# Clustered attention and two MLPs in one kernel: clusters of one pair of heads at a time, chosen amid attention

## Chip, cores and metric

One core of a Trainium2 chip runs the whole program. The metric is the device time of one execution in microseconds (us). Engines: TensorE (PE, its weight loads PEld), VectorE (DVE), ScalarE (ACT), GpSimd (POOL); SyncE (SP) and ACT issue DMAs.

## What is computed

```python
q_n, k_n, c_n = q / |q|, k / |k|, centroids / |centroids|     # (2, 8, 768, 64) and 8 heads x 16 clusters
q_assign = argmax(q_n @ c_n.T); k_assign = argmax(k_n @ c_n.T)   # first of equal maxima
mask = q_assign[..., :, None] == k_assign[..., None, :]
attn = softmax(where(mask, q @ k.T / 8, -1e9)) @ v
x = attn, heads side by side                                   # (1536, 512)
h = x @ w_in; g = h * sigmoid(1.702 * h); x = g @ w_out        # width 2048
h = x @ w_in2; s = h * softmax(h); x = layernorm(s) * g_ln @ w_out2   # width 1024
```

Length of q and k does not change an argmax, so only the centroids are normalized. The mask comes into the scores as 16 more rows of the contraction: a one-hot row set for q, and one times -2^100 for k, so that a query whose cluster differs from the key's gets a large negative term.

## The kernel before

Each engine has its own program; the order of its work is written by hand, and semaphores join the programs.

**Clusters** are found first, in 8 lots (2 batches x q or k x 2 halves of the 768 tokens, each lot all 8 heads). Per lot: `sims_of` (L446, four matmuls 128x32 weights by 384 columns, L453), `copy_sims` on ACT (L705), three transposes (`tokens_of`, L465), on DVE a maximum over 16 clusters and a comparison (`compare`, L919 and L921), on POOL a product with a falling rank, so that the first of equal maxima wins (`rank_lot`, L1244), and on DVE a second maximum and comparison (`choose`, L930 and L935). Two lots make one set of one-hot rows: six transposes back (`hots_of`, L476) and an ACT copy to `hot_t` (`store_clusters`, L715), which goes by DMA to `mask_rows` in HBM (L368, L719). Six lots are chosen and two sets turned back before attention; the rest falls into its first steps (`HOT_STEPS`, `STORE_STEPS`, `CHOOSE_STEPS`, L261).

**Attention** runs over 8 pairs of heads (`it`), 12 steps each (`n`, 6 tiles of 128 queries for each head of the pair). `place_head` (L323, SP) moves halves of a head's split k and q and its cluster rows (L336, two DMAs of 48 KB) into the tiles that scores read. Step n:

- PE: turn the probabilities of step n-6 (`turn`, L519, 6 transposes), scores of step n (`scores_of`, L502 and L506), and a part of a half head (`head_half`, L534: 12 matmuls per 3 steps, in parts of 3, 5 and 4; part 0 and 1 behind the scores, part 2 before them).
- ACT: copy of the turned halves (`turned_high`, L772, two), the exponential (`exps`, L761), and in some steps k_high (L728), a copy of the half head (`x_of_low_v`, L778) or xh (L784).
- DVE: row maximum (L959), two small ones on sums in even steps (L967, L973), `x_sum` (L986) every third step, `turned_low` (L979, two).
- POOL: scaling of probabilities (L1221), k_low (L1158) and splits of v and x.

The order of a step on PE and DVE, and the banks (PSUM has 8):

```python
TURN_LAG, HEAD_LAG, X_LAG = 5, 6, 9
def pt_bank(step, c): return banks[:, 4 + (2 * step + c) % 3, 0:HALF]   # turned halves: 3 banks in turn
head_out = banks[:, 7, 0:HALF]                                          # one bank for all half heads
pe.wait_ge(pt_low_done, 2 * g - 2 + c)                                  # turn, half c of turn g
if exists(it, n, CH, STEPS): pe.wait_ge(x_done, it * 4 + half)          # head_half, part 0
```

Scores use banks 0 to 3. The pair `it` = 0 is written out, the others are loops with register operands on all engines (`Fori`). Behind attention come the first MLP (PE L549 to L566), and the second (L639 to L672), which the change leaves alone.

Of the kernel before, what the change touches and what calls it, by code (L numbers as in the profile page):

```python
# [5 lines left out]
ALU = mybir.AluOpType  # L6
# [6 lines left out]
P = 128  # L13
# [3 lines left out]
def clustered_attention_two_mlps(nc, q_t, k_t, v_r, cent, w_gelu, w_ln, gains, out):  # L17
# [24 lines left out]
    assert HC == P and DM == BANK and QT % 2 == 0 and F2 == 2 * BANK and UNITS == 16  # L42
# [3 lines left out]
    mask_rows = nc.dram_tensor("mask_rows", (2, B, HC, S), F32, kind="Internal").ap()  # L46
    mask_heads = mask_rows.rearrange("x b (h c) s -> x (b h) c s", c=C)

    with ExitStack() as ctx:
# [26 lines left out]
        pair_t = [sb(f"pair_t{x}", [P, HP, S], F32, raw34, "right") for x in range(2)]  # L76
        sims_t = [sb(f"sims_t{x}", [P, S], F32, raw34, "right") for x in range(2)]
        raw34.close()
# [3 lines left out]
        first_rank_i = sb("first_rank_i", [P, C], I32, cluster)  # L82
        first_rank = sb("first_rank", [P, C], F32, cluster)
# [5 lines left out]
        LOTS = 4 * B  # L89
        CHOICE_LAG = 1  # L90
        RANKS = CHOICE_LAG + 2
        sims_max = [sb(f"sims_max{r}", [P, CH * H], F32, cluster) for r in range(RANKS)]
        rank_max = [sb(f"rank_max{r}", [P, CH * H], F32, cluster) for r in range(RANKS)]
        rank = [sb(f"rank{r}", [P, HALF], F32, cluster) for r in range(RANKS)]
        hot = [sb(f"hot{x}", [P, S], F32, cluster) for x in range(2)]
        hot_t = [sb(f"hot_t{x}", [P, S], F32, cluster) for x in range(2)]
# [47 lines left out]
        sims_t_ps = [banks[:, 2 * x:2 * x + 2, 0:HALF] for x in range(2)]  # L144
        sims = [banks[:, 4 + c, 0:HALF] for c in range(2)]
        hot_ps = banks[:, 6:8, 0:HALF]
# [3 lines left out]
        def pt_bank(step, c):  # L150
            return banks[:, 4 + (2 * step + c) % 3, 0:HALF]

        head_out = banks[:, 7, 0:HALF]
# [18 lines left out]
        pair_loaded = [two_sems(f"pair_loaded{x}_") for x in range(2)]  # L172
# [5 lines left out]
        ranked = sem("ranked")  # L178
        rank_max_done = sem("rank_max_done")
        hot_done = sem("hot_done")  # L180
        hot_ps_done = sem("hot_ps_done")
        hot_t_done = sem("hot_t_done")
        mask_stored = two_sems("mask_stored")
# [68 lines left out]
        TURN_LAG, HEAD_LAG, X_LAG = 5, 6, 9  # L252
# [8 lines left out]
        KQ_STEP, STORE_STEPS, HOT_STEPS, CHOOSE_STEPS = 0, (2, 4), (3, 5), (0, 1)  # L261
# [27 lines left out]
        def _(sp):  # L289
            sp.dma_start(c_raw[:], cent).then_inc(cent_loaded, 16)  # L290
            sp.dma_start(gains_sb[:], gains).then_inc(gains_loaded, 16)


            def load_pairs(e):
                b, x, c = e // 4, e // 2 % 2, e % 2
                if b > 0:

                    sp.wait_ge(sims_t_done, e - 3)
                half = slice(c * HALF, (c + 1) * HALF)
                sp.dma_start(pair_t[x][:, :, half], (q_pairs, k_pairs)[x][b][:, :, half]  # L300
                             ).then_inc(pair_loaded[x][c], 16)
# [21 lines left out]
            def place_head(it, j):  # L323
# [6 lines left out]
                def cluster_rows(dst, x):  # L330
                    src = mask_heads[x, bass.ds(h, 1)].rearrange("o c s -> (o c) s")
                    if isinstance(it, int) and it == 0 and j == 0:

                        sp.wait_ge(hot_t_done, x + 1)
                        src = hot_t[x][0:C, :]
                    sp.dma_start(dst.bitcast(F32), src).then_inc(qk_ready[j], 16)  # L336
# [4 lines left out]
                if isinstance(it, int) and it == 0 and j == 0:  # L341

                    load_pairs(LOTS - 1)
# [5 lines left out]

                sp.wait_ge(low_moved[j], (it + 1) * 16)  # L350
                for x, rows in enumerate((q_high[j], k_low[j])):
                    cluster_rows(rows[D:AUG, :], x)
# [13 lines left out]
            for x in range(2):  # L366
                sp.wait_ge(hot_t_done, x + 1)
                sp.dma_start(mask_rows[x, 0], hot_t[x][:]).then_inc(mask_stored[x], 16)  # L368
            for j in range(2):
                load_v(0, j)  # L370
            load_kq(1, 0)

            for x in range(2):
                sp.wait_ge(mask_stored[x], 16)
            place_head(0, 1)

            def place_turn(it, last=False):
                load_kq(it, 1)
                place_head(it, 0)
                load_v(it, 0)  # L380
                if not last:
                    load_kq(it + 1, 0)
                place_head(it, 1)
                load_v(it, 1)
                load_ln(it)


            sp.wait_ge(sims_done, LOTS)
            load_ln(0)

            for x in range(2):
                sp.wait_ge(mask_stored[x], 16 * B)
            with sp.Fori(1, ITS - 1) as it:
                place_turn(it)
            place_turn(ITS - 1, last=True)


# [40 lines left out]
        def _(pe):  # L438

            pe.wait_ge(gpsimd_consts, 4)  # L440
# [5 lines left out]
            def sims_of(e):  # L446
                b, x, c = e // 4, e // 2 % 2, e % 2
                pe.wait_ge(pair_loaded[x][c], (b + 1) * 16)
                if e >= 4:

                    pe.wait_ge(sims_t_copied, e - 3)
                for n in range(HP):
                    last = nc.tensor.matmul(sims_t_ps[x][n * 2 * C:(n + 1) * 2 * C, c, :], c_diag[:, n, :],  # L453
                                            pair_t[x][:, n, c * HALF:(c + 1) * HALF], start=True, stop=True)
                last.then_inc(sims_t_done, 1)

            def tokens_of(e):
                x, c = e // 2 % 2, e % 2
                pe.wait_ge(sims_t_copied, e + 1)
                if e >= 2:  # L460

                    pe.wait_ge(compared, e - 1)
                for i in range(CH):
                    t = c * CH + i
                    last = nc.tensor.transpose(sims[c][:, i * P:(i + 1) * P], sims_t[x][:, t * P:(t + 1) * P],  # L465
                                               ident[:])
                last.then_inc(sims_done, 1)


            def hots_of(g):  # L470
                pe.wait_ge(hot_done, (g + 1) * 2)
                if g >= 1:

                    pe.wait_ge(hot_t_done, g)
                for i in range(QT):
                    last = nc.tensor.transpose(hot_ps[:, i // CH, i % CH * P:(i % CH + 1) * P],  # L476
                                               hot[g % 2][:, i * P:(i + 1) * P], ident[:])
                last.then_inc(hot_ps_done, 1)

            for e in range(4):  # L480
                sims_of(e)
                if e >= 1:
                    tokens_of(e - 1)
# [836 lines left out]
```

## Time and profile before

| | |
|---|---|
| runs | 671.86, 672.01, 675.32 us (median 672.01) |
| profiled execution | 672.1 us, span 670.3 us, granted clock 0.986 |
| clusters until the first scores | 0 to 31.5 us |
| attention, pair 0 | 31.5 to about 58 us |
| attention, pairs 1 to 7 | 27.0 us each, to about 247 us |
| drain and first MLP | to about 540 us |
| second MLP | to 670 us |

The span is from the first to the last instruction; 1.8 us of the time lie around it. Engine rows give busy time; matmuls overlap, so a busy PE need not be at its peak. In a timeline an idle time in brackets stands with what ended it; the chain of waits is followed back from the last instruction, and "issue" in it is time for which the profile shows no wait.

### The profile page before, as it was taken

How to read it: one execution, taken by the hardware profiler on the slowest of the kernel's cores; microseconds unless marked ns; L12 is line 12 of the kernel's file. 1: busy time of each engine (PE TensorE's matmuls, PEld its weight loads, DVE VectorE, ACT ScalarE, POOL GpSimd, SP SyncE). 2: the span in 40 equal slices, each digit the busy share in tenths (PEclk: the TensorE clock that was granted, in tenths of full speed). 3: DMA queues.
4: the chain of work that ended last, by engine and by line, in shares of the span. 5: the costliest groups of instructions: out<-in, count | busy, mean ns of one | idle time of the engine just before them, and what ended most of it. 6: DMA issues, size and time to landing. Idle time of an engine off the chain costs nothing.

```text
span 670.3 us, 11572 instructions
## 1 busy us (share of the span) xinstructions
PE 639.0 (95%) x3281; PEld 537.8 (80%) x3281; DVE 434.5 (65%) x759; ACT 321.0 (48%) x641; POOL 419.7 (63%) x590
## 2 busy tenths in 40 slices
PE   5689999999999999999999999999999999999998
PEld 1369989898989888788877888788888878888886
DVE  3779999999999985666657667562222554545352
ACT  1279999999999984222232222132222243324232
POOL 2677788798888886888878888878886100000000
PEclk9779999999999999999999999999999999999999
DMA  8866544544544421232222222222231022112101
GB/s 284 245 185 154 159 120 112 143 122 126 143 112 137 130 92 64 72 113 87 104 94 93 90 99 94 94 95 94 94 106 51 29 82 77 52 60 78 63 16 47
DMA packets 39601, 70.52 MB, mean 105 GB/s; under 512 B 4256, under 2 KB 22688, under 8 KB 39584
## 3 DMA queue, kind: packets, MB, share of 16 engines
q1 hardware_dynamic: 37568, 66.38, 33.1%
q10 hardware_dynamic: 2016, 3.93, 1.6%
q8 instruction: 8, 0.13, 0.1%
q14 instruction: 9, 0.07, 0.0%
HBM read 46.60 MB, written 4.72 MB: 77 GB/s over the span
## 4 chain that ended last, share of the span: by engine, by line
PE 68%; ACT 10%; issue 9%; DVE 5%; DMA 4%; POOL 2%; DVEq 1%; SPq 1%; ACTq 0%; POOLq 0%
PE banks L534 6%; PE banks L549 6%; PE banks L551 6%; PE banks L550 6%; PE banks L564 6%; PE banks L566 6%; PE banks L565 5%; PE banks L639 5%; ACT probs L761 4%; PE banks L519 4%; PE banks L672 3%; PE banks L671 3%; PE banks L670 3%; ACT probs_th L772 3%; PE banks L642 2%
## 5 line engine op out<-in xcount | busy, mean ns | idle before, releaser
L979 DVE TENSOR_TENSOR probs_tl<-banks,probs_th 128x384 fp32r<-128x384 f32 x192 | 100.5, 547 | 11.7 <-ACT probs_th L772 9.4
L959 DVE TENSOR_REDUCE neg_max<-banks 128x1 f32<-128x768 f32 x96 | 91.3, 951 | 8.6 <-PE banks L506 6.6
L772 ACT CAST probs_th<-banks 128x384 fp32r<-128x384 f32 x192 | 83.0, 485 | 20.8 <-PE banks L519 19.5
L761 ACT ACTIVATE probs<-banks,neg_max 128x768 f32<-128x768 f32 x96 | 88.3, 920 | 7.1 <-DVE neg_max L959 7.0
L953 DVE TENSOR_TENSOR gl<-gate,gh 128x512 fp32r<-128x512 f32 x48 | 48.2, 1003 | 66.8 <-ACT gh L746 66.8
L1145 POOL TENSOR_TENSOR wait_scrap<-half_power 128x1 f32<-128x1 f32 x176 | 46.4, 264 | 67.1 <-PE banks L566 33.7
L1221 POOL TENSOR_SCALAR probs<-probs,row_inv 128x768 f32<-128x768 f32 x96 | 87.0, 907 | 0.0
L1284 POOL TENSOR_TENSOR stat<-stat,half_power 128x1 f32<-128x1 f32 x12 | 6.6, 549 | 127.5 <-DVE stat L1092 127.5
L519 PE MATMUL banks<-ident,probs 128*128 128x128 f32 x576 | 79.0, 273 | 1.3 <-ACT hot_t L715 1.3
L534 PE MATMUL banks<-probs_th,v_parts 128*128 128x384 f32 x192 | 70.4, 367 | 9.8 <-DVE x_sums L986 9.8
L746 ACT CAST gh<-gate 128x512 fp32r<-128x512 f32 x48 | 29.8, 621 | 101.1 <-PE banks L566 52.7
L549 PE MATMUL banks<-xh,uph 128*128 (+1 forms) x192 | 76.0, 396 | 0.4 <-POOL upl L1194 0.4
L564 PE MATMUL banks<-gh,downh 128*128 128x512 f32 x192 | 75.8, 395 | 0.2
L566 PE MATMUL banks<-gh,downl 128*128 128x512 f32 x192 | 75.3, 392 | 0.0
L551 PE MATMUL banks<-xh,upl 128*128 (+1 forms) x192 | 75.3, 392 | 0.0
L550 PE MATMUL banks<-xl,uph 128*128 (+1 forms) x192 | 75.1, 391 | 0.0
L565 PE MATMUL banks<-gl,downh 128*128 128x512 f32 x192 | 74.8, 390 | 0.0
L1204 POOL TENSOR_TENSOR downl<-gelu_raw,downh 128x512 fp32r<-128x512 f32 x48 | 71.4, 1488 | 4.0
L519 PEld LDWEIGHTS banks<-ident,probs 128*128 128x128 f32 x576 | 68.5, 140 | 5.7 <-ACT hot_t L715 1.6
L742 ACT ACTIVATE gate<-banks 128x512 f32<-128x512 f32 x48 | 28.7, 599 | 81.8 <-PE banks L551 57.0
L1194 POOL TENSOR_TENSOR upl<-gelu_raw,uph 128x512 fp32r<-128x512 f32 x48 | 62.7, 1306 | 4.0
L534 PE MATMUL banks<-probs_tl,v_parts 128*128 128x384 f32 x192 | 65.1, 339 | 0.0
(100 smaller groups left out, 1346.1 us busy)
## 6 DMA issues: line engine op xcount, KB each, us to landing
gelu_raw<-w_gelu SPq DMA_DIRECT2D x48, 512.0 KB, 3.3
ln_raw<-w_ln SPq DMA_DIRECT2D x8, 512.0 KB, 4.3
pair_t<-q_t SPq DMA_DIRECT2D x4, 768.0 KB, 7.3
pair_t<-k_t SPq DMA_DIRECT2D x4, 768.0 KB, 8.2
kq_raw<-k_t SPq DMA_DIRECT2D x16, 192.0 KB, 3.5
kq_raw<-q_t SPq DMA_DIRECT2D x16, 192.0 KB, 3.7
q_parts<-k_high SPq DMA_DIRECT2D x16, 192.0 KB, 2.6
q_high<-k_high SPq DMA_DIRECT2D x16, 192.0 KB, 3.0
```

Source lines behind the costliest of these rows:

```text
L519: last = nc.tensor.transpose(pt_bank(n, c)[:, t * P:(t + 1) * P], probs[:, n % NP, k * P:(k + 1) * P], ident[:])
L534: last = nc.tensor.matmul(head_out, v_parts[j][:, i // 2].rearrange("p two d -> p (two d)"), part[half % 2][:, i // 2, :], start=i == 0, s ...
L549: nc.tensor.matmul(hidden[u], uph[u][:, cols], xh[:, k, tok], start=k == 0, stop=False)
L550: nc.tensor.matmul(hidden[u], uph[u][:, cols], xl[:, k, tok], start=False, stop=False)
L551: last = nc.tensor.matmul(hidden[u], upl[u][:, cols], xh[:, k, tok], start=False, stop=k == KT - 1)
L564: nc.tensor.matmul(acc[d], downh[u][:, cols], gh[u][:], start=first, stop=False)
L565: nc.tensor.matmul(acc[d], downh[u][:, cols], gl[u][:], start=False, stop=False)
L566: last = nc.tensor.matmul(acc[d], downl[u][:, cols], gh[u][:], start=False, stop=end)
L761: nc.scalar.activation(probs[:, n % NP, :].rearrange("p (c t) -> p c t", c=2), scores[n % 2], ACT.Exp, bias=neg_max[:, n % NP:n % NP + 1], ...
L772: nc.scalar.copy(probs_th[half % 2][:, c * CH:(c + 1) * CH, i * P:(i + 1) * P], pt_bank(n, c).rearrange("p (t s) -> p t s", t=CH)).then_in ...
L959: nc.vector.tensor_reduce(out=neg_max[:, col], in_=scores[n % 2], op=ALU.max, axis=mybir.AxisListType.XY, negate=True).then_inc(max_done, 1)
L979: nc.vector.tensor_tensor(probs_tl[half % 2][at], pt_bank(n, c).rearrange("p (t s) -> p t s", t=CH), probs_th[half % 2][at].bitcast(F32), ...
```

## The change

There are 8 lots, one for each pair of heads: q and k, both halves of the tokens, in one matmul group of the same shape as before (4 x 2C rows). Lot 0 is made whole before attention, lot 1 half; its rest lies in steps 1 and 3 of pair 0. Lot e >= 2 lies in the 12 steps of pair e-2: sims at step 1, its transposes and `compare` at step 4, transposes back and `copy_ties` at step 7, the tie matmul and `choose` at step 10. POOL ranks nothing any more: a 128x128 matrix `first_w` (made once on POOL with two `affine_select` and two subtractions) is multiplied with the transposed comparison, and `choose` is one comparison of the product, from PSUM to `hot_t`. Nothing goes through HBM: `cluster_rows` is four DMAs of 24 KB per head out of `hot_t`.

The lots borrow the banks of the half heads (6 and 7; lot 1 uses 4 and 5). Turned halves get two banks in place of three, half heads two in place of one, with later waits; `X_LAG` is 10. `x_of_low_v` goes to the head of a step, ahead of `turned_high`, and so from steps 1, 4, 7, 10 to 2, 5, 8, 11; xh from 6 and 9 to 7 and 10. `gains` is loaded later. All attention loops are written out (`for` in place of `Fori`).

```diff
-        TURN_LAG, HEAD_LAG, X_LAG = 5, 6, 9
+        TURN_LAG, HEAD_LAG, X_LAG = 5, 6, 10
+        LOT_LEAD = 2
+        LOT_STEPS = [{"sims_t": 1, "sims": 4, "ties": 7, "first": 10}] * (LOTS - LOT_LEAD)
-            return banks[:, 4 + (2 * step + c) % 3, 0:HALF]
-        head_out = banks[:, 7, 0:HALF]
+        def pt_bank(c):
+            return banks[:, 4 + c, 0:HALF]
+        def head_out(half):
+            return banks[:, 6 + half % 2, 0:HALF]
+        LOT_UNITS = ("sims_t", "sims", "ties", "first")
+        def lot_bank(what, e):
+            w = LOT_UNITS.index(what) % 2
+            return banks[:, (5 - w if e == 1 else 6 + w), 0:HALF]
@@ SP
-                    sp.dma_start(dst.bitcast(F32), src).then_inc(qk_ready[j], 16)
+                def cluster_rows(rows, x):
+                    for c in range(2):
+                        at = (x * 2 + c) * 2 * C + j * C
+                        sp.dma_start(rows[D:AUG, c * HALF:(c + 1) * HALF].bitcast(F32), hot_t[it % 2][at:at + C, :]
+                                     ).then_inc(qk_ready[j], 16)
-            for e in range(4):
-                load_pairs(e)
+            load_pair(0)
             load_kq(0, 0)
-            for e in range(4, LOTS - 1):
-                load_pairs(e)
+            load_pair(1)
             load_kq(0, 1)
+            sp.dma_start(gains_sb[:], gains).then_inc(gains_loaded, 16)
             place_head(0, 0)
...
@@ PE
+            def sims_of(e):
+                for x in range(2):
+                    for c in range(2):
+                        n = x * 2 + c
+                        last = nc.tensor.matmul(dst[n * 2 * C:(n + 1) * 2 * C, :], c_diag[:, e % HP, :],
+                                                pair_t[x][:, e % 2, c * HALF:(c + 1) * HALF], start=True, stop=True)
+            def first_of(e):
...
+                nc.tensor.matmul(lot_bank("first", e), first_w[:], ties_t[:], start=True, stop=True
+                                 ).then_inc(first_done, 1)
-                    if exists(it, n, 2 - c, STEPS):
-                        pe.wait_ge(pt_low_done, 2 * g - 2 + c)
+                    if g >= 1:
+                        pe.wait_ge(pt_low_done, 2 * g - 1 + c)
-                    if exists(it, n, CH, STEPS):
-                        pe.wait_ge(x_done, it * 4 + half)
+                    if exists(it, n, 2 * CH, STEPS):
+                        pe.wait_ge(x_done, it * 4 + half - 1)
+                    read, count = lot_read(it * 4 + half)
+                    pe.wait_ge(read, count)
+                    if not drain:
+                        for what, of in zip(LOT_UNITS, (sims_of, tokens_of, ties_of, first_of)):
+                            for e in lot_at(it, n, what):
+                                of(e)
-            attention_turn(0)
-            with pe.Fori(1, ITS) as it:
+            for it in range(ITS):
                 attention_turn(it)
@@ ACT
+            def copy_ties(e):
+                act.wait_ge(ties_done, e + 1)
...
+                nc.scalar.copy(ties_t[:], lot_bank("ties", e)).then_inc(ties_t_copied, 1)
@@ DVE
+                nc.vector.tensor_tensor(heads(ties[:]), sim, sims_max[:].unsqueeze(2).to_broadcast([P, G, C]), ALU.is_ge
...
+                nc.vector.tensor_scalar(hot_t[e % 2][:], lot_bank("first", e), hot_from[:], hot_scale[:], ALU.is_ge,
+                                        ALU.mult).then_inc(hot_t_done, 1)
@@ POOL
-            X_SPLIT_STEPS = [QT + 3, QT + 4]
+            X_SPLIT_STEPS = [QT + 2, QT + 5]
-            for e in range(LOTS):
-                rank_lot(e)
+            scale_q(0, 0)
+            first_weights()
```

## Rows read from the trace of the kernel before

**Rows 1.** Busy time by stretch: us, PE, PEld, DVE, ACT, POOL, clock, DMA share, GB/s
```profile
0.00:31.50 31.50, 18.27 (x102) 6.78 (x102) 18.27 (x39) 7.37 (x12) 13.45 (x23) 0.88 0.85 260
31.50:45.70 14.20, 11.05 (x42) 9.34 (x42) 9.50 (x17) 8.37 (x16) 9.82 (x14) 0.66 0.82 229
...
99.50:126.50 27.00, 25.74 (x170) 24.04 (x169) 25.43 (x53) 24.93 (x58) 22.88 (x35) 1.00 0.48 129
```

**Rows 2.** Waits, 100 to 225 us: us in total, times, longest
```profile
PEld banks L534 <- DVE x_sums L986: 11.4, 18, 0.7
```

**Rows 3.** Chain of waits, 98 to 129 us: start, us, what
```profile
110.80 0.48 ACT x_sums L778
...
111.82 0.56 DVE x_sums L986
```

**Rows 4.** Timeline of PEld, 104 to 113 us: start, us, what
```profile
106.08 0.76 PEld L519 LDWEIGHTS banks<-ident,probs 128*128 128x128 f32 x6
...
108.31 0.75 PEld L519 LDWEIGHTS banks<-ident,probs 128*128 128x128 f32 x6
...
110.38 0.75 PEld L519 LDWEIGHTS banks<-ident,probs 128*128 128x128 f32 x6
...
112.43 0.19 PEld L534 LDWEIGHTS banks<-probs_th,v_parts 128*128 128x128 f32 x1 [0.68 <-DVE x_sums L986]
```

**Rows 5.** Timeline of ACT, 46 to 52 us, pair 0, two exponentials in a row
```profile
49.64 0.90 ACT L761 ACTIVATE probs<-banks,neg_max 128x768 f32<-128x768 f32 x1
...
51.43 0.90 ACT L761 ACTIVATE probs<-banks,neg_max 128x768 f32<-128x768 f32 x1
```

**Rows 6.** Timeline of DVE, 49 to 59 us, pair 0, three row maxima in a row
```profile
50.44 0.95 DVE L959 TENSOR_REDUCE neg_max<-banks 128x1 f32<-128x768 f32 x1
...
52.36 0.95 DVE L959 TENSOR_REDUCE neg_max<-banks 128x1 f32<-128x768 f32 x1
...
54.15 0.95 DVE L959 TENSOR_REDUCE neg_max<-banks 128x1 f32<-128x768 f32 x1
```

**Rows 7.** Timeline of ACT, 98 to 114 us, k_high and what follows it
```profile
99.42 0.84 ACT L728 CAST k_high<-kq_raw 128x768 fp32r<-128x768 f32 x1
100.15 0.88 ACT L772 CAST probs_th<-banks 128x384 fp32r<-128x384 f32 x2
```

**Rows 8.** Groups of instructions, 0 to 36 us: busy us, mean ns | idle before
```profile
L921 DVE TENSOR_TENSOR rank<-banks,sims_max 128x384 f32<-128x384 f32 x8 | 4.5, 558 | 0.3
L919 DVE TENSOR_REDUCE sims_max<-banks 128x24 f32<-128x384 f32 x8 | 4.4, 551 | 9.1 <-PE banks L465 9.1
L705 ACT COPY sims_t<-banks 128x384 f32<-128x384 f32 x8 | 3.8, 478 | 16.3 <-PE banks L453 16.3
...
L1158 POOL TENSOR_TENSOR k_low<-kq_raw,k_high 128x384 fp32r<-128x384 f32 x2 | 2.6, 1314 | 0.0
```

**Rows 9.** Timeline of PEld and PE, 22 to 26 us: a lot's matmuls behind transposes
```profile
24.35 0.16 PEld L453 LDWEIGHTS banks<-pair_t,c_diag 128*32 128x32 f32 x8 [0.17 <-issue]
...
24.35 0.85 PE L453 MATMUL banks<-pair_t,c_diag 128*32 128x384 f32 x8
```

**Rows 10.** Chain of waits over the span, first part: start, us, what
```profile
8.31 1.50 PE banks L453 x8
9.82 0.83 PE banks L465 x3
...
22.87 5.32 DMA q_parts<-k_low
...
28.83 2.62 DMA k_low<-hot_t
```

**Rows 11.** Timeline, 0 to 22 us: the first lot
```profile
6.30 1.51 PE L453 MATMUL banks<-pair_t,c_diag 128*32 128x384 f32 x8 [1.57 <-DMA pair_t<-q_t]
```

**Rows 12.** Timeline, 22 to 60 us: second head of pair 0
```profile
35.14 0.82 ACT L728 CAST k_high<-kq_raw 128x768 fp32r<-128x768 f32 x1
...
45.71 0.30 PEld L502 LDWEIGHTS banks<-k_high,q_parts 128*128 128x128 f32 x2 [1.25 <-DMA k_low<-mask_rows]
```

More of the change, by code:

```diff
@@ L384, in place_turn @@
                 load_v(it, 1)
+                if it + 3 < LOTS:
+                    load_pair(it + 3)
                 load_ln(it)
[L388 to L395, printed above, removed]
+            for j in range(2):
+                sp.wait_ge(qk_ready[j], READY * ITS)
             def gelu_turn(it):
@@ L438, in _ @@
         def _(pe):
[L440 removed]
+            pe.wait_ge(gpsimd_consts, 3)
             pe.wait_ge(cent_unit_done, 1)
@@ L446, in sims_of @@
             def sims_of(e):
[L447 to L454, printed above, removed]
+                pe.wait_ge(pair_loaded[e % 2], (e // 2 + 1) * 32)
@@ L802, in attention_turn @@
                             kq_high(0, 1)
-                        if n in STORE_STEPS:
-                            store_clusters(2 + STORE_STEPS.index(n))
+                    if not drain:
+                        for what, of in (("sims_t", copy_sims), ("ties", copy_ties)):
+                            for e in lot_at(it, n, what):
+                                of(e)
                     if drain and n in GATE_STEPS:
                         gelu(0, GATE_STEPS.index(n))
-            attention_turn(0)
-            with act.Fori(1, ITS - 1) as it:
-                attention_turn(it)
-            attention_turn(ITS - 1, last=True)
+            for it in range(ITS):
+                attention_turn(it, last=it == ITS - 1)
             attention_turn(ITS, X_STEPS[-1] + 1, drain=True)
@@ L939, in _ @@
-            for b in range(B):
-                for e in range(4 + CHOICE_LAG):
-                    if e < 4:
-                        compare(b * 4 + e)
-                    if e >= CHOICE_LAG and b * 4 + e - CHOICE_LAG < LOTS - len(CHOOSE_STEPS):
-                        choose(b * 4 + e - CHOICE_LAG)
+                dve.wait_ge(first_done, e + 1)
+                if e == 0:
+                    dve.wait_ge(hot_consts, 4)
+                if e >= 2:
+                    for j in range(2):
+                        dve.wait_ge(qk_ready[j], READY * (e - 1))
@@ L1007, in attention_turn @@
                         turned_low(*lagged(it, n, TURN_LAG, STEPS), 1)
+                    if not drain:
+                        for what, of in (("sims", compare), ("first", choose)):
+                            for e in lot_at(it, n, what):
+                                of(e)
                     if drain and n in GATE_STEPS:
@@ L1011, in _ @@
             dve.wait_ge(guard_set, 1)
-            attention_turn(0)
-            with dve.Fori(1, ITS) as it:
+            for it in range(ITS):
                 attention_turn(it)
```

299 lines of the change are left out of this document (137 added, 162 removed).

## The prediction

> **What bounds the kernel now.** I read the busy table by stretch first, since clusters, attention and MLPs have different limits. [rows 1] show three stretches that the change touches: 31.5 us until the first scores, 14.2 us from there to the scores of the second head, and laps of 27.0 us for a pair. In a lap PE is busy 25.7 us, DVE 25.4 and ACT 24.9, so no engine has much room, and what ends a wait decides. The waits say which: PE's weight loads stood 11.4 us in 18 waits, all for x_sum [rows 2], and 125 us are 4.63 laps, so 2.5 us a lap, four waits of 0.6. The chain shows the loop behind it: the half head's copy on ACT, x_sum on DVE, then the next half head on PE [rows 3, 4]. There is one bank for half heads, so each must be emptied before the next begins.
>
> In the first stretch the chain [rows 10] runs over DMAs: moving k_low took 5.3 us among the big pair loads, the cluster rows 2.6 more.
>
> **Part 1, up to the first scores.** All 8 lots' loads stood in front; now only 0.79 MB (pair 0's q and k) come first. The first load landed at 6.3 us before [rows 11], itself 0.79 MB; I take 6.0. Then at the slow clock: sims 1.5, copy 0.5, transposes 0.8, compare 1.15, transposes 0.8, copy 0.5, tie matmul 0.5 (one matmul of their 384 columns, between one transpose's 0.3 and the 0.8 of all three), choose 0.56 [rows 8, 10, 11]: 12.3 us. Choose has no row: a plain comparison of its size took 0.56 [rows 8]; its bounds are 0.48, a copy's, and 1.1, compare's two together.
>
> Beside it k and q of head 0 land at about 7.5 (1.18 MB at 260 GB/s, [rows 1], behind an issue at 1.2, plus the landing); scaling and k_high end near 10. On POOL `first_weights` now stands ahead of k_low: four operations of 128 columns or less, for which no row stands; by width a third of k_low's 1.3 [rows 8] is 0.45 each, 1.8 in all; between nothing and 4 x 1.3 = 5.2. With 1.2 to 1.8 and two k_low of 1.3, k_low is ready at about 12.9. Its move takes 2.6 to 5.3 [rows 10]; the pair loads are then through, so 2.6: 15.5. SP then issues two DMAs of cluster rows, 0.6, and they land 2.6 later: first scores at 18.7, against 31.5. Gain 12.8, between 10 and 14.
>
> **Part 2, second head of pair 0.** Its k_high comes behind the first exponential on ACT, as before, at 35.14, and the scores waited for the cluster rows until 45.71 [rows 12]: 10.6 us for k_low, moves and rows. That order stays; what goes is the store to HBM and back and the DMA load of the other lots, what comes is two more issues on SP. I take 9.3, gain 1.3, between -1 and 3.
>
> **Part 3, cost of a lot in a lap.** PE: sims, of the shape they had, took 0.85 at the fast clock, with 0.17 idle ahead [rows 9]: 1.02 in step 1. Three transposes at half of six's 0.7 [rows 4] are 0.35 in step 4 and in step 7; the tie matmul is taken at 0.18, half of those, in step 10. Sum 1.9. The 0.17 is a row: weight loads of 32 columns waited for transposes of 128, and nothing is named but issue. The Trainium skill (TensorEngine Tiling (Array Packing), Key Properties) says that a change of tiling mode drains TensorE. The row agrees. A lot changes the mode twice; by this rule 0.17 more would be paid on the way back, 1 us over six lots. ACT: two copies of 0.48 [rows 8], steps 1 and 7. DVE: compare 1.15 in step 4, choose 0.56 in step 10.
>
> **Part 4, the lap.** Step lengths of one engine without waits: ACT 1.79 [rows 5]; DVE 1.79, and 1.92 in even steps [rows 6]; PE 2.23, 2.07 and, less its stall of 0.68, about 1.9 [rows 4]. Extras: k_high 0.73 [rows 7], a half-head copy or an xh 0.48, x_sum 0.5 [rows 3]. Sums over 12 steps before: PE 24.8, DVE 24.2, ACT 25.8. Taking the longest engine in each step and adding gives 27.3, and the lap took 27.0: steps are coupled nearly rigidly.
>
> After, PE has 26.7, DVE 25.9, ACT 26.8: no lap with a lot can be under 26.8. The longest engine per step, 0 to 11, is 2.4 (DVE), 3.25 (PE), 2.3, 2.3, 3.1 (DVE with compare), 3.0 (ACT: k_high and the half-head copy now meet in 5 and 11), 2.4, 2.75 (ACT), 2.3, 2.3, 2.5, 3.0: 31.5. That is the upper bound. Two banks for turned halves make PE's turn wait for DVE's `turned_low` of the turn just before. That loop takes turn 0.7, copy 0.5, subtraction 0.55, about 1.75, so a step forgives some 0.4 us. Walking turn by turn with this (turn begins at the latest of PE's own step, and 1.05 behind the ACT copy's start; the copy at the latest of turn plus 0.5 to 0.7, and ACT's last work; DVE in its order) puts the turns of steps 0 to 12 at 0, 1.9, 5.1, 7.2, 9.4, 12.0, 14.0, 16.7, 19.3, 21.4, 24.0, 26.4, 28.5, and the lap carries 0.4 into the next: 28.9. Without a lot the same walk gives 26.3: the old wait on x_sum goes, but ACT's 25.8 is close behind.
>
> Who waits behind the new waits: in steps 3, 6, 9 and 0 part 0 of a half head stands on PE until the lot has left its bank; the walk has the lot out 0.2 to 0.6 us ahead. Compare delays row maximum 5 and so exponential 5; late next is ACT.
>
> At nothing: pair loads amid attention (DMA share 0.48 a lap [rows 1], some 0.6 after), four more small issues on SP a lap, `gains`. If that cover were gone, scores would wait at steps 0 and 6. The written-out loops I also take at nothing.
>
> **Sum**, against the profiled execution's 672.1 (the median is the same within 0.1): -12.8 - 1.3; pair 0's lots 1 and 2 among its steps +1.1; pairs 1 to 5, 5 x (28.9 - 27.0) = +9.5; pairs 6 and 7, 2 x (26.3 - 27.0) = -1.4; x_sum one step later in the drain +0.3. Together -4.6: 667.5 us.
>
> **Rivals.**
> (a) *The lots hide in the old stall.* The stall of 2.5 us a lap was as large as PE's 1.9, and ACT and DVE have the room by their sums. Laps of 27.0 with a lot, 25.9 without: -12.8 - 1.3 + 0.5 - 2.2 + 0.3 gives 656.6. For it: every sum is under 27. Against it: steps 1, 4, 5 and 11 each load one engine 3 us, and two banks leave little to even that out.
> (b) *Slower: the two-bank loop holds the steps rigidly.* The place is PE's turn waiting for `turned_low`, above all behind compare and sims. The lap then nears 31.5, and gain and loss meet where it is 27.0 + 14.1 / 5 = 29.8. At 30.5 with 27.5 for pairs 6 and 7 it gives -12.8 - 1.3 + 1.6 + 17.5 + 1 + 0.3: 678.4. For it: 27.3 against 27.0 before, though then with three banks. Against it: the 0.4 us of slack.
> (c) *Pair 0 runs late.* The clock was 0.66 between the first scores and the second head's [rows 1], at times at 1.2 GHz, and PE has less to do ahead of scores now; a slow clock for some 6 us more in full steps costs 3, a late second head 1 to 2: 671.5.
> (d) *It doesn't remove what it seems to:* the half-head bank was one of two equal waits, so pairs 6 and 7 stay at 27.0. That is +1.4, 669, and stands in (c)'s range.
>
> **Numbers.** Forecast 0.40, (a) 0.23, (b) 0.19, (c) and (d) 0.18. This kernel's measurement tells about 0.5% (3.4 us) from nothing. Faster by more than that (under 668.6): a good half of the forecast, 0.26, all of (a), 0.03 of (c) and (d): 0.52. Slower (over 675.4): most of (b), 0.18, and 0.02 of (c): 0.20. The same: 0.28. The range 656 to 678 takes in (a) and the lower half of (b).
>
> **What would show it.** First scores at 18 to 20 us; second head's some 13 us behind them; laps with a lot of 28.2 to 29.6 and without of 26 to 26.6; in place of PE waiting for x_sum, PE at L519 waiting for `turned_low`, most in steps 2 to 3 and 6 to 7. It is wrong if laps 1 to 5 stay near 27, if they pass 30, or if first scores come after 21.

## The result, and the profile after

| | before | after |
|---|---|---|
| runs, median | 671.93 us (671.83 to 675.32) | 676.91 us (676.27 to 677.69) |
| profiled execution, span | 672.1, 670.3 us | 677.22, 675.5 us |
| first scores | 31.50 us | 17.96 us |
| first scores of the second head, behind the first | 14.2 | 12.35 |
| first scores of pair 1, behind those | 11.8 | 16.22 |
| laps of pairs 1 to 5 | 26.42, then 27.0 to 27.2 | 30.65, then 29.58 four times |
| lap of pair 6 (no lot) | 27.00 | 27.10 |
| pair 7 to the first matmul of the MLP | 31.88 | 32.18 |
| from there to the end | 419.2 | 420.7 |

The ratio is 1.0066, 95% interval 1.0039 to 1.0093: slower, if by little. 15.4 us came in until the second head and 20.6 us went out behind it. The same table of stretches as [rows 1], of the kernel after:

```profile
0.00:17.96 17.96, 6.73 (x27) 2.36 (x27) 4.44 (x19) 3.55 (x5) 6.77 (x20) 1.00 0.68 184
17.96:30.31 12.35, 9.87 (x45) 7.45 (x45) 7.12 (x13) 7.04 (x15) 6.37 (x10) 1.00 0.69 184
30.31:46.53 16.22, 12.09 (x77) 10.30 (x77) 13.42 (x28) 13.90 (x31) 13.55 (x21) 1.00 0.67 174
46.53:52.00 5.47, 5.47 (x26) 5.13 (x30) 3.62 (x7) 1.85 (x4) 2.11 (x4) 0.69 0.65 177
77.20:106.80 29.60, 27.82 (x187) 24.74 (x184) 26.83 (x57) 26.02 (x59) 22.94 (x35) 1.00 0.57 145
195.50:222.60 27.10, 26.48 (x171) 23.74 (x170) 25.67 (x54) 25.34 (x57) 22.97 (x35) 1.00 0.45 115
```

The clock column is not to be read before 24.1 us: the profile has no clock record there, and the durations say that PE was slow (sims took 1.51 at 21.3 us and 0.85 in the laps; the first scores 1.01, those at 26.65 us 0.62).

A lap with a lot keeps PE busy 27.8 us of 29.6, one without 26.5 of 27.1. The waits between 100 and 225 us show that the wait for x_sum of [rows 2] is gone, and which waits stand now:

```profile
ACT probs_th L778 <- PE banks L534: 10.9, 16, 0.9
DVE probs_tl L978 <- ACT probs_th L778: 7.9, 15, 0.8
PE banks L534 <- DVE probs_tl L978: 6.8, 16, 0.7
```

L534 is now the turn, L778 its copy on ACT, L978 the subtraction on DVE (`turned_low`). Beside them PE's weight loads stand 14.3 us ahead of turns, and the profile names no wait for that. PE, ACT and DVE stand for one another in turn: a ring in which the work of each comes behind that of the last. The chain of waits through a lap with a lot (pair 2; start, us, what) goes round it:

```profile
80.56 0.89 PE banks L551 x5
81.45 0.78 PE banks L458 x8
...
84.50 0.37 ACT sims_t L719
...
84.89 0.26 ACT x_sums L784
...
85.39 0.49 ACT probs_th L778
...
85.90 0.57 DVE probs_tl L978
...
86.60 0.98 PE banks L534 x6
...
89.16 0.33 PE banks L469 x3
...
91.45 0.47 DVE sims_max L921
...
91.95 0.56 DVE ties L926
92.50 0.87 DVE neg_max L958
...
96.50 0.33 PE banks L479 x3
...
99.35 0.30 ACT ties_t L727
```

Every piece of the lot but choose stands in this chain: sims 0.78 and its copy 0.37, transposes 0.33, compare 1.03, transposes 0.33, copy 0.30, and the tie matmul (0.17, at 104.02). That is 3.3 us, and the lap is 2.5 longer than one without a lot: some of it is covered, and a piece in the chain is not yet a price.

**Ahead of pair 1** the loss has another cause. SP's timeline there, with PE's below it:

```profile
29.67 0.43 SPq L314 DMA_DIRECT2D pair_t<-q_t  x1
30.14 0.43 SPq L314 DMA_DIRECT2D pair_t<-k_t  x1
30.62 0.43 SPq L367 DMA_DIRECT2D ln_raw<-w_ln  x1
31.09 0.51 SPq L324 DMA_DIRECT2D kq_raw<-k_t  x1
31.65 0.60 SPq L324 DMA_DIRECT2D kq_raw<-q_t  x1
32.57 0.90 SPq L342 DMA_DIRECT2D q_parts<-k_high  x1
33.51 0.70 SPq L342 DMA_DIRECT2D q_high<-k_high  x1
35.74 0.46 SPq L342 DMA_DIRECT2D q_parts<-k_low  x1
42.17 0.46 SPq L342 DMA_DIRECT2D k_high<-k_high  x1
```

```profile
46.53 0.62 PE L515 MATMUL banks<-k_high,q_parts 128*128 128x384 f32 x2 [3.53 <-DMA k_low<-hot_t]
...
48.93 0.99 PE L515 MATMUL banks<-k_high,q_parts 128*128 128x384 f32 x2
```

Within 2.6 us SP issued a pair load, the `ln` load and k and q of the next head, 1.66 MB, and right behind them pair 1's moves of k_high. Those were issued at 32.6 and 33.5 and landed 7.4 and 8.6 us later, and SP's next step, which waits for them, came at 42.17. PE stood 3.5 us for the cluster rows behind it. 1.4 us after it had started again it fell to 1.2 GHz for 3.4 us: the same scores take 0.99 in place of 0.62, and the granted clock is 0.69 from 46.5 to 52.0. The Trainium skill (DMA: Bandwidth & Descriptors, Queues, rings and completion order) says that each DMA engine takes a queue's descriptors in ring order; moves issued behind 1.66 MB of loads landed 8.6 us behind their issue here in place of 3.0, which agrees.

### The profile page after: what moved, and what is told of

Read it like the earlier page. It is cut to its first block, busy times and chain, and to the rows that moved or that the text cites. A ratio compares the mean times of both kernels' runs of the same rounds, so it can differ in the third digit from the quotient of the medians.

```text
span 675.5 us, 10622 instructions
## 1 busy us (share of the span) xinstructions
PE 641.4 (95%) x3289; PEld 535.7 (79%) x3289; DVE 424.8 (63%) x754; ACT 323.0 (48%) x645; POOL 412.3 (61%) x586
## 4 chain that ended last, share of the span: by engine, by line
PE 74%; ACT 8%; DVE 7%; issue 5%; DMA 2%; POOL 2%; SPq 1%; POOLq 0%; DVEq 0%; ACTq 0%
PE banks L534 7%; PE banks L566 6%; PE banks L654 6%; PE banks L568 6%; PE banks L581 6%; PE banks L567 6%; PE banks L583 6%; PE banks L582 6%; PE banks L551 5%; PE banks L686 3%; PE banks L687 3%; PE banks L685 3%; ACT probs_th L778 3%; DVE probs_tl L978 3%; PE banks L657 3%
## 5 line engine op out<-in xcount | busy, mean ns | idle before, releaser
L978 DVE TENSOR_TENSOR probs_tl<-banks,probs_th 128x384 fp32r<-128x384 f32 x192 | 100.6, 548 | 20.6 <-ACT probs_th L778 19.5
L778 ACT CAST probs_th<-banks 128x384 fp32r<-128x384 f32 x192 | 85.0, 483 | 30.3 <-PE banks L534 29.2
L534 PE MATMUL banks<-ident,probs 128*128 128x128 f32 x576 | 85.8, 282 | 11.8 <-DVE probs_tl L978 11.5
L534 PEld LDWEIGHTS banks<-ident,probs 128*128 128x128 f32 x576 | 63.9, 141 | 33.8 <-issue 25.2
L952 DVE TENSOR_TENSOR gl<-gate,gh 128x512 fp32r<-128x512 f32 x48 | 46.1, 960 | 69.6 <-ACT gh L752 69.6
L752 ACT CAST gh<-gate 128x512 fp32r<-128x512 f32 x48 | 29.8, 621 | 102.2 <-PE banks L583 57.4
L551 PE MATMUL banks<-probs_th,v_parts 128*128 128x384 f32 x192 | 67.9, 353 | 0.0
```

What stands on the lines that cost most here:

```text
L534: last = nc.tensor.transpose(dst[:, t * P:(t + 1) * P], probs[:, n % NP, k * P:(k + 1) * P], ident[:])
L551: last = nc.tensor.matmul(head_out(half), v_parts[j][:, i // 2].rearrange("p two d -> p (two d)"), part[half % 2][:, i // 2, :], start=i = ...
L778: nc.scalar.copy(probs_th[half % 2][:, c * CH:(c + 1) * CH, i * P:(i + 1) * P], pt_bank(c).rearrange("p (t s) -> p t s", t=CH)).then_inc(p ...
L978: nc.vector.tensor_tensor(probs_tl[half % 2][at], pt_bank(c).rearrange("p (t s) -> p t s", t=CH), probs_th[half % 2][at].bitcast(F32), ALU ...
```

## Experiments

Each is one run, and stands beside runs of the kernel before (medians of 672.9 to 673.7 us, where the result above has 671.93) unless an interval is given; so I read laps first, and the whole time only where it moves by more than 2 us. "Later loads" is `new_loads_later` below, from which most of the later kernels start.

**1. Where the bound lay before.** Three parts of the change alone, or undone.

`old_written_out`: the loops alone, on all five engines.

```diff
-            with pe.Fori(1, ITS) as it:
+            for it in range(1, ITS):
```

> The kernel before with its attention loops written out, nothing else. Theory (loops cost nothing): laps stay at 27.0 us, time 672 within 1. Rival (branches and register waits cost): laps 26.5 or less, time under 668. Other rival (code loading costs in straight code): over 674.

672.21 us, laps 27.01 to 27.03. Writing the loops out costs and gives nothing.

`old_two_two`: the same, with the change's banks.

```diff
-            return banks[:, 4 + (2 * step + c) % 3, 0:HALF]
-
-        head_out = banks[:, 7, 0:HALF]
+            return banks[:, 4 + c, 0:HALF]
+
+        def head_out(half):
+            return banks[:, 6 + half % 2, 0:HALF]
...
-                    if exists(it, n, 2 - c, STEPS):
-                        pe.wait_ge(pt_low_done, 2 * g - 2 + c)
+                    if exists(it, n, 1, STEPS):
+                        pe.wait_ge(pt_low_done, 2 * g - 1 + c)
...
-                    if exists(it, n, CH, STEPS):
+                    if exists(it, n, 2 * CH, STEPS):
...
-                        pe.wait_ge(x_done, it * 4 + half)
+                        pe.wait_ge(x_done, it * 4 + half - 1)
```

> The kernel before, written out, with two banks for turned halves and two for half heads, the order of work unchanged (X_LAG 9, half-head copy behind the exponential). Theory 1 (the bank split only moves the wait from x_sum to turned_low): laps 26.8 to 27.3. Theory 2 (it is the new place of the half-head copy that holds the pairs without a lot at 27.1; the split by itself frees the wait): laps 25.8 to 26.5, time 664 to 668.

673.49 us, laps 27.20: theory 1. PE's wait for x_sum is gone. In the kernel before it had two rows between 100 and 225 us, the weight loads' in [rows 2] (11.4 us) and the matmuls' own, half as long, since matmuls are still at work while the next weights wait:

```profile
PE banks L534 <- DVE x_sums L986: 5.7, 18, 0.4
```

In `old_two_two` this stands in its place:

```profile
PE banks L520 <- DVE probs_tl L980: 6.2, 18, 0.5
```

The wait has moved, the lap has not shrunk. And PE never stood 2.5 us a lap: 5.7 us in 4.63 laps are 1.2. The last of this group takes only the part that can hurt, two banks for turned halves and still one for half heads:

`old_two_one`: of the diff above only `pt_bank` and the wait for `pt_low_done`.

> The kernel before with written-out loops (672.21 us, laps 27.0), two banks in turn for turned halves in place of three, and still one for half heads: the half of the bank split that can cost. Theory G (give and take: the second half-head bank gives what the missing third turned bank takes, which is why the lap without a lot stayed at 27.1 where a gain was forecast): without the second half-head bank both waits stand, PE for x_sum before part 0 and PE for turned_low one step later; laps 27.6 to 28.6, 677 to 683 us. Theory E (the engines' own work sets 27.0, banks of either kind don't matter): 27.0 to 27.3, 672 to 674 us.

Laps 27.28. In all 678.33 us, a time of G's range and not of E's, but its first scores came at 33.6, 2.1 later than before, and pair 0 took 1.0 more; only the laps are read. By them theory E's number holds, and G, on which I had come to rely, falls. Its two waits do not even add up: PE stands for x_sum as before, and for `turned_low` only weight loads stand, 0.8 us in all.

```profile
PE banks L534 <- DVE x_sums L986: 6.3, 18, 0.4
```

With or without either bank, a lap without a lot takes 27.0 to 27.3, and PE stands 1.2 to 1.4 us in it.

**2. Pair 1.** `new_loads_later`: the kernel after with two loads later.

```diff
             load_v(0, 1)
-            load_pair(3)
-            load_ln(0)
             for it in range(1, ITS):
                 load_kq(it, 1)
                 place_head(it, 0)
                 load_v(it, 0)
+                if it == 1:
+                    load_pair(3)
+                    load_ln(0)
```

> The changed kernel with pair 3's load and the first weight load of the second MLP issued behind the moves of head 0 of pair 1. Theory 1 (1.3 MB of loads ahead of those moves made them late and PE stood 3.5 us before pair 1, then ran at half clock): scores of pair 1 begin at 43 or earlier in place of 46.5, time 672 to 674. Theory 2 (ACT and POOL are late with k_high and k_low for that head): the wait stays, time 676 to 677.

671.74 us: pair 1's first scores stood 11.8 behind the second head's, as before the change. Its lap 1 was still 30.66: PE waited 0.66 us for the pair load that is now issued later (sims in step 1), and its weight loads 0.35 and 0.55 for the cluster rows of the next two heads. The same edit with an interval, as `new_loads_timed`:

> The kernel after with nothing but the two loads moved behind pair 1's first moves, against before with an interval: 670.5 to 673.5 us, ratio 0.997 to 1.001. Against after's 676.9 that is the 5 us which stood in PE's wait for the cluster rows and the slow clock behind it; if it is over 675, the one look was luck and the loads are not the cause.

Here lap 1 was 29.37, and the clock stayed at 1.00 from 23.5 us on. 672.32 us (671.06 to 673.69, 9 runs), 0.998 of before, 95% interval 0.9969 to 0.9991. Its SP timeline has the k_high moves landed by 36.07, 3.2 us behind their issue:

```profile
32.92 0.60 SPq L342 DMA_DIRECT2D q_high<-k_high  x1
35.56 0.46 SPq L342 DMA_DIRECT2D q_parts<-k_low  x1
36.07 0.60 SPq L342 DMA_DIRECT2D k_high<-k_high  x1
```

So the change's net loss lay in the place of 1.28 MB of loads. What is left is a balance near zero: 15 us gained ahead, 13 lost in laps 1 to 5, the rest in the last two pairs and the drain.

**3. What a lot costs in a lap.** All but `new_x_behind` on top of the later loads (laps 29.57, and 27.10 without a lot).

`new_one_sim`:

```diff
                         n = x * 2 + c
+                        if e >= LOT_LEAD and n != 3:
+                            continue
```

> The kernel after with the later loads; of the four sims matmuls of each lot from the third on, only the last is left (the other rows of the lot are not computed). PE gets 0.6 us less in step 1. Theory R: in step 1 PE's own work (turn, scores, five matmuls of the half head, sims) is the longest path round, so the whole 0.6 comes off the lap: 28.9 to 29.0. Theory S as well for this step. If the lap stays at 29.4 or more, the turn behind sims waits for DVE anyway and PE's extra work is not what a lot costs; then 671 us. With the 0.6: 668.4 to 668.9 us.

672.02 us, laps 29.52, where 668.4 to 668.9 and 28.9 to 29.0 were expected. The expectation was wrong about PE: one matmul took as long as four. The sims in this kernel, and in the kernel after:

```profile
105.86 0.83 PE L461 MATMUL banks<-pair_t,c_diag 128*32 128x384 f32 x2
```
```profile
110.96 0.85 PE L458 MATMUL banks<-pair_t,c_diag 128*32 128x384 f32 x8
```

The four go to four different groups of 32 columns, and 0.85 for four beside 0.83 for one says that they run side by side. The Trainium skill (TensorEngine Tiling (Array Packing), Key Properties) says that different tiles can execute in parallel; these rows agree.

`new_no_sims`: all four left out.

```diff
                             for e in lot_at(it, n, what):
-                                of(e)
+                                if what != "sims_t":
+                                    of(e)
...
-                act.wait_ge(sims_t_done, e + 1)
+                act.wait_ge(sims_t_done, min(e + 1, LOT_LEAD))
```

> The kernel after with the later loads; all four sims matmuls of each lot from the third on are left out (the copy takes what stands in the bank, so these lots are not computed). One matmul or four took the same time on PE, 0.85, since the four go to different columns of the array side by side; so the run that left one in took away nothing. Theory P (in steps 1 and 2 PE has no idle time, its own work is the path): with none left step 1 is shorter by the 0.74 between sims and the turn behind them and by the 0.17 to 0.25 of idle time ahead: 3.0 to 3.2 in place of 3.94, laps with a lot 28.6 to 28.8, 666.5 to 668 us. Theory D (DVE or ACT hold step 1): laps above 29.3, 671 us or more.

668.29 us; in the steady laps step 1 takes 3.22 in place of 3.94 to 3.97, as it does without a lot, and step 3 2.45 in place of 2.50; laps 28.78. Theory P.

`new_no_compare`: the same on DVE.

```diff
-                pe.wait_ge(compared, e + 1)
+                pe.wait_ge(compared, min(e + 1, LOT_LEAD))
...
-                                of(e)
+                                if what != "sims" or e < LOT_LEAD:
+                                    of(e)
```

> The kernel after with the later loads; DVE's compare (maximum and comparison, 1.03 us) is left out of each lot from the third on, so these lots turn back the comparison of an earlier one. Theory R: compare stands in front of row maximum 5, so it comes off almost whole, less what PE's transposes of the lot in step 4 hold: laps 28.7 to 29.0, 667.5 to 669 us. Theory S (PE is the bound behind step 4): 29.3 or more, 670.5 to 671.5 us. With the one sim of the run before this splits the 2.5 us of a lot; what is left over by both, 0.8 to 1, is the transposes, the copies and choose.

667.92 us; step 6 2.07 in place of 2.71, no other changed, laps 28.90 to 28.93. Theory R. The two prices, 0.79 and 0.66, are those of the two pieces alone; compare itself lasts 1.03, so 0.37 of it was covered. From the steps' lengths (with a lot less without) the rest is 0.42 in step 3, 0.30 in step 4 and 0.38 in step 9. By their place these are the sims' copy, the transposes and the ties' copy, but no run took them out one by one. Together 2.5; nothing is left for choose.

`new_x_behind`: the half head's copy on ACT behind the exponential of the step before, as it had been, on top of the kernel after (676.91 us, laps 29.58).

```diff
-TURN_LAG, HEAD_LAG, X_LAG = 5, 6, 10
+TURN_LAG, HEAD_LAG, X_LAG = 5, 6, 9
...
-                        x_of_low_v(*lagged(it, n, X_LAG - 1, STEPS))
...
                     if not drain:
                         exps(it, n)
...
+                        x_of_low_v(*lagged(it, n, X_LAG - 1, STEPS))
```

> The changed kernel with the half-head copy back behind the exponential (steps 1, 4, 7, 10) and X_LAG 9. Theory 1 (the copy ahead of turned_high stands in the loop turn, ACT copy, subtraction, turn, and costs 0.3 to 0.5 each): laps with a lot 28.0 to 28.8 in place of 29.6, pair 6 26.3 or less, the drain 1 us shorter, time 669 to 673. Theory 2 (the lot's work sets the lap): laps 29.4 to 29.7, time 675 to 677.

679.67 us, laps 30.23 to 30.30 with a lot, 27.61 without, against both theories: the new place is the better one. Most of the loss stands in step 6, 3.42 in place of 2.71, where PE waited 1.3 us for `turned_low` and its weight loads for POOL's scaled probabilities. Why these came late there stays open. The next moves the other end of the half head, x_sum on DVE.

`new_x_sum_last`:

```diff
-                        x_sum(*lagged(it, n, X_LAG, STEPS))
...
                         turned_low(*lagged(it, n, TURN_LAG, STEPS), 0)
...
                         turned_low(*lagged(it, n, TURN_LAG, STEPS), 1)
...
+                        x_sum(*lagged(it, n, X_LAG, STEPS))
```

> The kernel after with the later loads (671.74 us, laps with a lot 29.57, without 27.10) and on DVE x_sum moved behind both turned_low of its step. Theory R (a ring: turn and scores on PE, row maximum and then turned_low on DVE, and only then the next turn; what stands on DVE between row maximum and turned_low counts whole): the step that follows each x_sum (steps 0, 3, 6, 9 hold one, 0.5 us each) gets up to 0.5 shorter where PE had waited for turned_low 0.3 to 0.65; laps with a lot 28.2 to 28.8, without 26.0 to 26.6, in all 663 to 666 us. Theory S (the engines' own work in a step sets it, DVE has the same work wherever x_sum stands): laps 29.4 to 29.7 and 27.0 to 27.2, 671.5 us.

687.59 us, laps 32.5 with a lot and 27.84 without: my largest miss, of the wrong sign. PE in step 1:

```profile
113.11 0.85 PE L459 MATMUL banks<-pair_t,c_diag 128*32 128x384 f32 x8 [0.86 <-DVE x_sums L987]
```

The lot's pieces live in the half heads' banks. A piece can't start until x_sum has emptied the bank, and all that stands behind it on PE waits with it. The banks are not the whole of it, since laps without a lot lost 0.7 too. The bank is as tight at its other end:

`new_compare_split`:

```diff
-                        for what, of in (("sims", compare), ("first", choose)):
+                        for what, of in (("sims", sims_top), ("first", choose)):
                             for e in lot_at(it, n, what):
                                 of(e)
+                        if n >= 1:
+                            for e in lot_at(it, n - 1, "sims"):
+                                compare(e)
```

> The kernel after with the later loads and compare in two: its maximum (0.47) stays at the end of DVE's step 4, its comparison (0.56) goes to the end of step 5. Theory R: row maximum 5 comes 0.56 earlier and with it turned_low and turn 6; row maximum 6 comes 0.56 later in a step where DVE waits for nothing either, so the step behind step 4 gives 0.3 to 0.5 back and the next takes 0 to 0.3: laps 29.2 to 29.4, 670 to 671 us. Theory S: DVE's sum is the same and its full steps only change place: 29.5 to 29.7, 671.5 us or a little more.

676.49 us, laps 30.37 to 30.41, against both theories. Part 0 of a half head waited for the lot to leave the bank:

```profile
120.81 0.41 PE L552 MATMUL banks<-probs_th,v_parts 128*128 128x384 f32 x1 [1.42 <-DVE ties L930]
```

`new_x_between`:

```diff
+                        turned_high(*lagged(it, n, TURN_LAG, STEPS), (0,))
...
                         x_of_low_v(*lagged(it, n, X_LAG - 1, STEPS))
...
-                        turned_high(*lagged(it, n, TURN_LAG, STEPS))
...
+                        turned_high(*lagged(it, n, TURN_LAG, STEPS), (1,))
```

> The kernel after with the later loads; on ACT the copy of the half head stands between the two turned copies of its step (c = 0 before it, c = 1 behind it) in place of ahead of both. The turn on PE in steps 1, 4, 7, 10 waits 0.3 to 0.65 for turned_low of c = 0, which stands behind this ACT copy of 0.48 and, in step 2, the copy of the lot. Theory A (ACT's order makes that wait): it goes for c = 0 and comes back in part for c = 1, 0.1 to 0.3 a step: laps 28.6 to 29.2, 667 to 670 us. Theory B (the bank: whatever delays x_sum delays the lot's piece a step later): x_sum stands ahead of turned_low on DVE and now waits longer itself, so the lap gains nothing or loses 0.1 to 0.4: 29.6 to 30.0, 672 to 674 us.

673.42 us: laps 29.3 with a lot, 0.27 less, but 27.65 without, 0.55 more. Theory A's sign holds for laps with a lot and theory B's for laps without; neither foretold both, and in all nothing is won.

**4. A version that beats both.** PE stands for turned_low behind the steps with three matmuls of a half head, and not at all where five and a piece of the lot meet.

`new_split_534`: later loads, and

```diff
-        UP_STEPS, GATE_STEPS = (2, 5), (5, 7)
+        UP_STEPS, GATE_STEPS = (2, 5), (6, 7)
...
-            HEAD_SPLIT = (0, 3, 8, 12)
+            HEAD_SPLIT = (0, 5, 8, 12)
```

> The kernel after with the later loads; a half head's twelve matmuls go in parts of 5, 3 and 4 in place of 3, 5 and 4, and in the drain the first gate of the MLP stands in step 6 in place of 5, behind x_sum. Theory P: PE stands 0.3 to 0.65 for turned_low behind the part of three, in four steps of a lap, and has no idle time in the steps with five and a piece of the lot. Two matmuls (0.35) moved from the full step to the one with the gap fit into the gap: 0.25 to 0.35 off each, 1.0 to 1.4 a lap: laps with a lot 28.2 to 28.6, without 25.9 to 26.3; the drain gives back about 1. In all 661 to 665 us, 0.983 to 0.990 of the kernel before. Theory D (the ring over ACT and DVE holds the lap): the gap moves to the other step, laps 29.3 to 29.7 and 27.0, 670.5 us. Against both: part 0 starts in the bank that the lot has to leave, and five matmuls there change nothing of that.

668.96 us (667.34 to 672.27, 4 runs), 0.9934 of before, 0.9915 to 0.9953. The profiled execution is its slowest, 672.27: laps 1 to 3 took 31.4, 30.3 and 29.7, with a wait of 2.3 us for cluster rows ahead of pair 2 and 1.2 GHz for 3.4 us right behind it. Its steady laps took 28.8 to 28.9: 0.7 off, where 1.0 to 1.4 were expected. That came off steps 1 and 4 alone; steps 7 and 10 kept their 3.4 and 3.3. Laps without a lot took 27.02, where theory P had 25.9 to 26.3 and D had 27.0: so P's gap was there to be filled only in part, and for laps without a lot D holds. From the first matmul of the MLP to the end it took 419.4, so most of the drain's loss is back. The control is the split in the kernel before:

`old_split_534`

> The kernel before with written-out loops and a half head's matmuls in parts of 5, 3, 4. There PE's idle time stands ahead of part 0, for x_sum, 0.6 to 0.7 in four steps, and not ahead of the turn behind it. Theory G and P: nothing moves into a gap, since the gap is ahead of part 0; laps 26.9 to 27.3, 671 to 675 us. If the laps fall below 26.8 the split is a gain of its own that has nothing to do with the change.

Laps 27.01 to 27.04 (673.92 us in all): nothing there. The split repairs something of the laps with a lot alone.

`new_rows_early`: the same as `new_split_534`, with

```diff
                 move(q_high[j][low, :], k_high[j][high, :], high_moved[j])
+                if it >= 1:
+                    sp.wait_ge(hot_t_done, it + 1)
+                    cluster_rows(q_high[j], 0)
                 sp.wait_ge(kq_low_done, (h + 1) * 2)
...
-                sp.wait_ge(hot_t_done, it + 1)
-                cluster_rows(q_high[j], 0)
+                if it == 0:
+                    sp.wait_ge(hot_t_done, it + 1)
+                    cluster_rows(q_high[j], 0)
```

> The later loads, the parts 5, 3, 4, the gate behind x_sum in the drain, and from pair 1 on q's cluster rows issued ahead of SP's wait for k_low, not behind the move of k_high (1.23 us of SP less at the end of the chain). The version without the last of these ran between 667.3 and 672.3 us, and in its slowest run PE waited 2.3 us once and 0.5 once for the cluster rows at the head of a pair. If that wait is what spread it: no wait on the rows over 0.3, laps with a lot 28.7 to 28.9 throughout, first scores of pair 1 up to 1.2 earlier; 665 to 668 us, 0.988 to 0.993 of before. If the spread comes from elsewhere: 667 to 671.

**668.18 us** (667.32 to 670.55, 6 runs), 0.9921 of before, 95% interval 0.9906 to 0.9937. That is clear of `new_loads_timed` (0.9969 to 0.9991, in the same session). Laps 28.92 throughout (28.75 the first), and between 60 and 250 us PE's waits have a single row:

```profile
PE banks L539 <- DVE probs_tl L983: 5.8, 22, 0.6
```

In the profiled execution of `new_split_534`, its slowest, there were 2.8 us for the cluster rows beside it. Five of the six runs lie within 1.0 us of each other, but the median lies in the range of the second case (667 to 671) and the intervals of the two versions overlap; what the earlier rows are worth by themselves stays open.

## Why the prediction was wrong

Forecast 667.5, measured 676.91; the range (to 678) held it, at the far end, but the forecast was a gain and the measurement is a loss. Two steps failed: the pair loads amid attention, put at nothing, and PE's own work in the walk of part 4. By the forecast's own terms, in the two profiled executions:

| term | forecast | measured |
|---|---|---|
| first scores | -12.8 | -13.5 |
| second head | -1.3 | -1.9 |
| pair 1's first scores (lots 1, 2 among pair 0's steps) | +1.1 | +4.5 |
| pairs 1 to 5 | +9.5 | +14.3 |
| pairs 6 and 7 | -1.4 | +0.4 |
| drain, to the end | +0.3 | +1.5 |
| sum | -4.6 | +5.2 |

- **Part 1 and 2 held, part 1 with luck.** Moves and cluster rows set first scores, and the lot itself was not on the path (its rows stood ready at 13.5 us, forecast 12.3). But the chain goes over k and q of head 0, whose q landed at 7.99, over the move of k_high (3.0) and over SP's issues of the rows, four and not two: 2.5 us from 14.17 in place of 0.6. The forecast had k_low's move and its landing at 15.5 in their place. The two errors nearly cancel.
- **"At nothing: pair loads amid attention" failed.** I had read the DMA share of a lap, 0.48, and priced the loads by it. What counts is what is queued when a move is issued: 1.66 MB in a burst ahead of pair 1's moves. This cost 3.5 us of PE's wait, and the 1.1 that lap 1 took above the others behind it (all of it in step 1, at the slow clock). Issuing two of the loads later gave 5.2 us back in `new_loads_later` and 4.6 by the medians in `new_loads_timed`. The forecast named the sign of it ("scores would wait at steps 0 and 6") and gave it no price.
- **The walk's base was too short.** Part 4 had 28.9 with a lot and 26.3 without, a difference of 2.6; measured 29.58 and 27.10, a difference of 2.5. So the lot's price was right as a sum (the walk names no price by piece, so whether its parts were right is not shown), and the lap under it 0.7 to 0.8 too low in all seven laps: with the 1.1 of lap 1 that is nearly the whole miss of pairs 1 to 7 (6.6 us). The term at fault is PE's own work, taken as 24.8 a lap. It comes from "2.23, 2.07 and, less its stall of 0.68, about 1.9" [rows 4], and 0.68 is the stall of the weight loads. PE's matmuls stood half of that at the same place:

```profile
112.43 0.44 PE L534 MATMUL banks<-probs_th,v_parts 128*128 128x384 f32 x1 [0.36 <-DVE x_sums L986]
```

With its own waits, 1.2 us a lap, PE's work is 27.0 less 1.2, so 25.8, and [rows 1] had it busy 25.7. In pair 6 the chain stays on PE without a wait for three whole steps:

```profile
203.89 0.86 PE banks L534 x6
204.75 0.35 PE banks L515 x2
205.10 0.36 PE banks L519 x2
205.46 0.89 PE banks L551 x5
206.35 0.66 PE banks L534 x6
207.00 0.70 PE banks L551 x4
207.70 0.35 PE banks L515 x2
208.05 0.35 PE banks L519 x2
208.40 0.66 PE banks L534 x6
209.05 0.35 PE banks L515 x2
209.40 0.35 PE banks L519 x2
209.75 0.53 PE banks L551 x3
210.28 0.84 PE banks L534 x6
```

From 203.89 to 210.28 are 6.39 us, so 25.6 a lap with nothing to wait for. A lap of 26.3 would have left the ring 0.7 us in twelve steps. It took 1.5 in pair 6, whose other groups of three steps lasted 6.7 to 7.1 us, and 1.2 in the kernel before. What the walk gives with PE's longer steps was not worked out. The 0.17 us that part 3 thought of on the way back from sims does not show: PE's turn starts 0.78 behind the start of sims, with no idle time between.
- **The 2.5 us of waits for x_sum were no reserve.** The forecast took that the old wait "goes" and ACT is next; `old_two_two` and `old_two_one` show that with this wait or without it the lap is the same within 0.3. The wait that takes its place is that of the ring; why the ring closes at 27.0 to 27.3, and not lower, is not shown.
- **The drain** lost 1.2 more than forecast: an x_sum came behind the MLP's first gate on DVE (265.95 us, behind 265.23), not only a step later. With the gate one step later, in `new_split_534` and `new_rows_early`, the stretch went from 420.5 (`new_loads_timed`) to 419.4.
- **The rivals.** (d) was right for pairs 6 and 7. (c) was half right: the clock was slow until 24.1 us, but the second head was not late, and pair 1 was, through the loads. (b) named the place, PE's turn waiting for `turned_low`, and its break-even, 29.8 a lap, is where the laps came to lie (mean 29.8), but its price (30.5 and 27.5) was too high; the sign was reached through pair 1, which no rival had. (a) is refuted: of the lot only choose and 0.8 of the 3.3 us in the chain hid.

## What to carry to other kernels

A stall is not a reserve until an experiment has taken it away: the bank that removed it only handed the wait to the next member of a ring, and of 3.3 us of work put into that ring 2.5 showed. Before idle time of the weight loads is counted, look at the row of the matmuls for the same wait: here it was half. Before a transfer is called hidden, list what is queued ahead of the next move that someone waits for; the mean DMA share of a lap, 0.48, did not show it. And when work borrows a buffer between two uses, both neighbours become deadlines: pieces can be moved by less than a step.

## What the hardware showed that I had not expected

- One 128x32 matmul of 384 columns takes PE 0.83 us, four into different column groups 0.85 together.
- A wait of 3.5 us on PE was followed by 3.4 us at 1.2 GHz (0.69 granted from 46.5 to 52.0), and so was one of 2.3 us in `new_split_534` (0.64 granted from 74.2 to 79.0). A wait of 1.4 in `new_loads_timed` left it at 1.00.
- Moves of 192 KB within the chip's own memory landed 2.6 to 3.0 us behind their issue by the median, and 7.4 and 8.6 us behind it with 1.66 MB just ahead in the queue.
